# Attention beside early expert tiles: masked queries behind the residual, root between the scatter halves, leaf columns shared anew, keys loaded by quarters, and the last early tile's outputs in three banks

## What is computed

```
attention, per batch and head, over 768 steps t (head_dim 48):
    y[t]   = q[t] @ state
    state += beta[t] * outer(k_n[t], v[t] - k_n[t] @ state)      k_n = k / (|k| + 1e-6)
first expert layer, x of 3072 x 384, 8 experts of 1024:
    P = exp(logits - max), 8 rounds of row and column normalisation
    out += P[:, e] * (relu(x @ w1[e]) @ w2[e])     for every e, all tokens
second layer, 384 -> 2048 -> 384:
    h = x @ w_in;  out = (h * cos(h)) @ w_out
```

## Time and profile before

| | us |
|---|---|
| median of 3 runs | 2282.24 |
| lowest, highest | 2277.13, 2284.86 |
| the profiled execution's own time | 2282.22 |
| its span, first to last instruction | 2280.5 |
| TensorE's mean granted clock | 0.981 |
| attention and early tiles, up to the first matmul of L612 | 393.4 |

### The profile page before, as it was taken

How to read it: one execution, slowest core, us unless ns; L and a number is a source line. 1 busy time by engine, 2 the same in 40 slices (tenths; PEclk the granted TensorE clock), 3 DMA queues, 4 the chain that set the end, 5 groups by cost and what they waited for, 6 DMA issues and landing times.

```text
span 2280.5 us, 40218 instructions
## 1 busy us (share of the span) xinstructions
PE 2222.2 (97%) x15494; PEld 1846.7 (81%) x15494; DVE 1023.6 (45%) x1744; ACT 721.2 (32%) x1153; POOL 508.3 (22%) x404
## 2 busy tenths in 40 slices
PE   4899998999999999999999999999999999999999
PEld 4788786888888888888888888888888888888887
DVE  7787732642222232323232323232323247777777
ACT  4555543311111111111111111111111126666665
POOL 1000001005433333332323232323232331000000
PEclk6799999999999999999999999999999999999999
DMA  5334233202110111111111010111010110000001
GB/s 121 86 86 114 72 102 102 70 16 61 33 32 28 39 35 32 28 32 28 38 35 32 28 32 28 31 42 32 28 33 28 34 36 15 14 14 15 0 15 69
DMA packets 81705, 97.68 MB, mean 43 GB/s; under 512 B 5632, under 2 KB 67392, under 8 KB 81600
## 3 DMA queue, kind: packets, MB, share of 16 engines
q1 hardware_dynamic: 81600, 96.18, 15.7%
HBM read 82.69 MB, written 8.75 MB: 40 GB/s over the span
## 4 chain that ended last, share of the span: by engine, by line
PE 82%; DVE 1%; ACT 0%; issue 0%; DVEq 0%
PE h L612 7%; PE h L613 7%; PE h L614 7%; PE p_h L612 7%; PE p_h L613 7%; PE p_h L614 7%; PE am_y L647 4%; PE am_y L648 4%; PE am_y L649 4%; PE chain_y L647 2%; PE chain_y L648 2%; PE chain_y L649 2%; PE o_y L647 2%; PE state_y L647 2%; PE o_y L648 2%; PE state_y L648 2%
## 5 line engine op out<-in xcount | busy, mean ns | idle before, releaser
L1137 POOL TENSOR_TENSOR acc<-acc,py 128x512 f32 (+1 forms) x252 | 324.3, 1319 | 747.0 <-DVE py L1439 747.0
L1002 ACT ACTIVATE hhi<-h 128x512 fp32r<-128x512 f32 x182 | 109.0, 599 | 769.5 <-PE h L614 769.5
L1402 DVE SCALAR_TENSOR_TENSOR hlo<-h,hhi 128x512 fp32r<-128x512 f32 x182 | 125.9, 692 | 474.6 <-ACT hhi L1002 474.6
L1402 DVE SCALAR_TENSOR_TENSOR hlo<-p_h,hhi 128x512 fp32r<-128x512 f32 x182 | 125.9, 692 | 404.5 <-ACT hhi L1002 404.5
L1099 POOL TENSOR_TENSOR wlo<-stage,whi (+1 forms) x114 | 148.5, 1304 | 652.1 <-ACT whi L881 626.1
L612 PE MATMUL p_h<-xhi,whi 128*128 (+1 forms) x690 | 268.8, 390 | 0.6 <-DVE scr L1499 0.6
L612 PE MATMUL h<-xhi,whi 128*128 (+1 forms) x690 | 268.7, 389 | 0.0
L613 PE MATMUL p_h<-xlo,whi 128*128 (+1 forms) x690 | 268.5, 389 | 0.0
L613 PE MATMUL h<-xlo,whi 128*128 (+1 forms) x690 | 268.4, 389 | 0.0
L614 PE MATMUL p_h<-xhi,wlo 128*128 (+1 forms) x690 | 268.4, 389 | 0.0
L614 PE MATMUL h<-xhi,wlo 128*128 (+1 forms) x690 | 268.4, 389 | 0.0
(11 more groups left out here) (240 smaller groups left out, 3996.7 us busy)
## 6 DMA issues: line engine op xcount, KB each, us to landing
stage<-wcat SPq DMA_DIRECT2D x38, 768.0 KB, 4.3
pb<-p_scratch SPq DMA_DIRECT2D x84, 256.0 KB, 4.7
kq<-kqt SPq DMA_DIRECT2D x48, 192.0 KB, 3.5
kT<-kta SPq DMA_DIRECT2D x24, 192.0 KB, 4.6
v<-vrow SPq DMA_DIRECT2D x24, 192.0 KB, 4.3
kb<-krow SPq DMA_DIRECT2D x24, 192.0 KB, 4.8
acc<-yT SPq DMA_DIRECT2D x72, 64.0 KB, 2.8
acc<-y_scratch SPq DMA_DIRECT2D x5, 768.0 KB, 4.7
```

Of the source, the lines that this page charges most:

```text
L1002: act.activation(hhi[:, j, :], hps[j % 2][:, 0:TILE], ACT.Relu).then_inc(s["hhi_done"], 1)
L1137: pool.tensor_tensor(y, y, py[:, d, :], ALU.add).then_inc(s["added"], 1)
L1402: dve.scalar_tensor_tensor(out=hlo[:, j, :], in0=hps[j % 2][:, 0:TILE], scalar=0.0, in1=hhi[:, j, :].bitcast(F32), op0=ALU.max, op1=ALU.su ...
```

## The change

- `masked(i)` moves from step i-1 to step i, directly behind `residual(i)`. At c=2 and c=3 the leaf and early work is ordered anew: norms and leaf_init of group g+2 come before `early_lo(g-1, 2)`, values of the next step behind it. Columns in steps c=0, 1, 3 change from 12..21 (two lists), 22..30, 1..11 to 10..20, 21..30, 1..9; in group 0 from 4..15, 16..30 (with 1..3 ahead of the loop) to 1..16, 17..30.
- The first three `first_w_lo` move from (g=1, c=0) to (g=1, c=1).
- ACT: `root(g + 2)` is issued between the two halves of `scatter(g + 1, 0)` instead of behind `merged`; scatter walks its elements in the order of the source instead of that of the destination.
- Keys of group 0: eight DMAs of a quarter each, with a semaphore per quarter, in place of four of a half.
- PE prologue: 8 warm matmuls instead of 3; 16 unread matmuls, ahead of the merges, once the leaf chain of group 0 has reached column 27; the waits for zeroed, gate_lo and consts behind the merges.
- DVE prologue: the mask copies ahead of the first extracts; values, masked and the gate's low part behind leaf_end.
- Tail: outputs of tile 4 go to am_ps[0], am_ps[1] and chain_ps; the first of them stands ahead of the logits; `x_hi(NT - 1)` stands ahead of `early_logits(4)` on ACT; `early_lo(4, 3)` ahead of `x_lo(0)` on DVE; the last gate waits for the logits' evacuation only, and the RAW tile's first down product for all of tile 4's.

The diff, cut to its core:

```diff
-COLS = {0: ((12, 14), (14, 22)), 1: ((22, 24), (24, L - 1)), 3: ((), (1, 12))}
-FIRST_COLS = {0: ((4, 7), (7, 16)), 1: ((16, 18), (18, L - 1))}
+COLS = {0: (10, 21), 1: (21, L - 1), 3: (1, 10)}
+FIRST_COLS = {0: (1, 17), 1: (17, L - 1)}
+NEAR_END = 2 + 1 + 2 * 26
...
+    def early_bank(t, d):
+        return (*am_ps, chain_ps)[d] if t == EARLY - 1 else o_ps
...
+        def first_kT(r):
+            for b in range(2):
+                n = slice(r * RU, (r + 1) * RU)
+                at_half = slice(r % 2 * RU * CT, (r % 2 + 1) * RU * CT)
+                sp.dma_start(kT[b * CT:b * CT + HD, n, :].rearrange("p n i -> p (n i)"),
+                             kta[0, r // 2, b, :, at_half]).then_inc(a[f"kt_first{r}"], 16)
...
-        load_kT(0, 0)
-        load_kT(0, 1)
+        for r in range(4):
+            first_kT(r)
...
-            pe.wait_ge(o["evac"], OUTS * t)
+            pe.wait_ge(o["evac"], OUTS * t if t < EARLY else OUTS * (t - 1) + 2)
...
-            pe.wait_ge(o["evac"], OUTS * t + 2 + d)
+            if t < EARLY - 1:
+                pe.wait_ge(o["evac"], OUTS * t + 2 + d)
+            elif d < 2:
+                pe.wait_ge(a["m_evac"], 4 * NG)
+            else:
+                pe.wait_ge(a["w_evac"], NS)
+            bank = early_bank(t, d)
...
-        for _ in range(3):
+        for _ in range(8):
             pe.matmul(p_ps[:, 0:2 * P], stage[:, 0:P], stage[:, P:3 * P], start=True, stop=True)
...
         query_products(0)
+        pe.wait_ge(a["a_evac"], 4)
+        pe.wait_ge(s["whi_done"], 1)
+        pe.wait_ge(a["leaf_chain"], NEAR_END)
+        unread(16)
         for m in range(3):
             merge(0, m)
...
         early_gate(t)
+        early_down(t, 0)
         early_logits(t)
-        for d in range(DC):
-            early_down(t, d)
+        early_down(t, 1)
+        early_down(t, 2)
...
+                if mode == RAW and j == 0:
+                    pe.wait_ge(o["evac"], OUTS * EARLY)
...
-                act.activation(X[L * q:L * q + L, g % 2, n, f:f + L], z_x[L * q:L * q + L, :, n].rearrange("p i n -> p n i"),
+                act.activation(X[L * q:L * q + L, g % 2, n, f:f + L].rearrange("p n i -> p i n"), z_x[L * q:L * q + L, :, n],
...
                 if c >= 2 and near:
-                    scatter(g + 1, c - 2)
+                    scatter(g + 1, c - 2, 0, 2)
+                    if c == 2 and far:
+                        root(g + 2)
+                    scatter(g + 1, c - 2, 2, 4)
                     merged(g + 1, 2 * (c - 2))
-                if c == 2 and far:
-                    root(g + 2)
...
         early_gate(t)
+        x_hi(NT - 1)
         early_logits(t)
         for d in range(DC):
             early_out(t, d)
-        x_hi(NT - 1)
```

More of the change, by code:

```diff
@@ L474, in early_down @@
                 pe.wait_ge(s["wlo_done"], NT)
-            pe.wait_ge(o["evac"], OUTS * t + 2 + d)
+            if t < EARLY - 1:
[5 more added lines that the diff above has]
+            bank = early_bank(t, d)
             for j in range(CH):
-                pe.matmul(o_ps[:, :], w2(whi, 0, j, d), hhi[:, j, :], start=(j == 0), stop=False)
-                pe.matmul(o_ps[:, :], w2(whi, 0, j, d), hlo[:, j, :], start=False, stop=False)
-                mm = pe.matmul(o_ps[:, :], w2(wlo, 0, j, d), hhi[:, j, :], start=False, stop=(j == CH - 1))
+                pe.matmul(bank[:, :], w2(whi, 0, j, d), hhi[:, j, :], start=(j == 0), stop=False)
+                pe.matmul(bank[:, :], w2(whi, 0, j, d), hlo[:, j, :], start=False, stop=False)
+                mm = pe.matmul(bank[:, :], w2(wlo, 0, j, d), hhi[:, j, :], start=False, stop=(j == CH - 1))
             mm.then_inc(o["down_done"], 1)
@@ L586, in _ @@
         pe.wait_ge(a["zeroed"], 2)
-        pe.wait_ge(a["a_evac"], 4)
-        pe.wait_ge(s["whi_done"], 1)
         pe.wait_ge(s["gate_lo"], 1)
@@ L874, in early_out @@
                     act.wait_ge(a["z_done"], NG)
-            act.activation(y_stage(t)[:, d, :], o_ps[:, :], ACT.Copy).then_inc(o["evac"], 1)
+            act.activation(y_stage(t)[:, d, :], early_bank(t, d)[:, :], ACT.Copy).then_inc(o["evac"], 1)
         def split_hi(buf, chunk, p, part=None, came=stage):
@@ L1289, in _ @@
             dve.memset(bank[:, :], 0.0).then_inc(a["zeroed"], 1)
+        dve.wait_ge(a["masks"], 1)
+        for b in range(2):
+            dve.tensor_copy(mask[b * CT:(b + 1) * CT, :], mask_all[b * CT:(b + 1) * CT, b * CT:(b + 1) * CT]).then_inc(a["mask_cut"], 1)
         first_extract(1)
@@ L1294, in _ @@
         leaf_init(0)
-        leaf(1, 12)
+        leaf(1, 28)
+        assert count[0] == NEAR_END
+        leaf(28, L - 1)
+        leaf_end(0)
         values(0)
-        dve.wait_ge(a["masks"], 1)
-        for b in range(2):
-            dve.tensor_copy(mask[b * CT:(b + 1) * CT, :], mask_all[b * CT:(b + 1) * CT, b * CT:(b + 1) * CT]).then_inc(a["mask_cut"], 1)
+        leaf_start(1)
+        dve.wait_ge(a["mask_cut"], 2)
+        masked(0)
+        norms(1)
+        leaf_init(1)
         dve.wait_ge(s["gate_hi"], 1)
@@ L1302, in _ @@
                           ALU.subtract).then_inc(s["gate_lo"], 1)
-        leaf(12, L - 1)
-        leaf_end(0)
-        dve.wait_ge(a["mask_cut"], 2)
-        masked(0)
-        leaf_start(1)
-        norms(1)
-        leaf_init(1)
-        leaf(1, 4)
         for g in range(NG):
@@ L1314, in _ @@
                 i = g * STEPS + c
-                cols = FIRST_COLS if g == 0 and c < 2 else COLS
                 residual(g, c)
-                if c == 2 and g >= 1:
-                    early_x_lo(g - 1)
-                if c == 2 and near:
-                    leaf_end(g + 1)
-                values(i + 1)
+                if i > 0:
+                    masked(i)
                 if c == 0 and g >= 2:
                     early_lo(g - 2, 3)
-                if c == 3 and g >= 1:
-                    early_lo(g - 1, 1)
-                if near and c < 2:
-                    leaf(*cols[c][0])
-                masked(i + 1)
-                if near and c < 2:
-                    leaf(*cols[c][1])
-                if c == 0 and g in (1, 2):
-                    for chunk in range((g - 1) * NT // 2, g * NT // 2):
-                        first_w_lo(chunk)
                 if c == 2:
                     if g >= 1:
+                        early_x_lo(g - 1)
+                    if near:
+                        leaf_end(g + 1)
+                    if g >= 1:
                         early_lo(g - 1, 0)
-                    if far:
-                        leaf_start(g + 2)
                 if c == 3:
                     if g >= 1:
-                        early_lo(g - 1, 2)
+                        early_lo(g - 1, 1)
                     if far:
@@ L1344, in _ @@
                         leaf_init(g + 2)
-                        leaf(*COLS[c][1])
+                    if g >= 1:
+                        early_lo(g - 1, 2)
+                values(i + 1)
+                if c == 2 and far:
+                    leaf_start(g + 2)
+                if near and c < 2:
+                    leaf(*(COLS if g else FIRST_COLS)[c])
+                if far and c == 3:
+                    leaf(*COLS[c])
+                if g == 1 and c == 1 or g == 2 and c == 0:
+                    for chunk in range((g - 1) * NT // 2, g * NT // 2):
+                        first_w_lo(chunk)
+        early_lo(EARLY - 1, 3)
         x_lo(0)
-        early_lo(EARLY - 1, 3)
         x_lo(NT - 1)
```

8 lines of the change are left out of this document (5 added, 3 removed).

## The result

The changed kernel takes 2254.65 us (median of 4 runs, 2252.70 to 2257.68) against 2279.68 (4 runs, 2276.27 to 2284.86) for the kernel before beside it: a ratio of 0.9889, 95% interval 0.9865 to 0.9914. The profiled execution took 2254.29. The prediction was 2255.5, with a range of 2248 to 2266.

A forecast was written before the change was run, and what follows sets the result against it. The prediction took the kernel as PE-bound (busy 97% of 2280.5 us), with the slow clock behind waits as second cost. Ten terms summed to -26.8 us, from a median of 2282.24 to 2255.5, range 2248 to 2266.

The forecast's parts named there:

- Term 1: Prologue: 1.0 us of work leaves DVE's chain, the first transpose comes 0.35 us later: -0.7 us.
- Terms 2 and 3: Step 2: idle for R 1.0 instead of 2.67 us (-1.7); full clock, less 0.6 for z_done (-2.5).
- Rival (b): DVE bounds groups 0 and 1, waits drop the clock, masked shows in two steps: 2262 us, chance 0.21.
- Terms 4 and 5: Step 4: the wait of 3.84 us goes (-3.84) and the step runs at full clock (-3.4).
- The falls behind merges: As many clock falls behind small-matmul merges as before, at 92, 157 and 311 us, some 1.5 us each.
- Rival (a): Unread matmuls carry the clock through step 0, two or three merge falls stay out: 2250 us, chance 0.17.
- Term 6: Steps 4 to 6: small waits as DVE and PE run abreast, 0.5 at step 6's merge: +0.5 us in all.
- Term 7: Step 8's wait of 1.30 us goes; early_down at step 9 waits 1.0 for first_w_lo: -0.3 us.
- Term 8: Step 12's masked comes 0.1 us late; the wait of 0.64 at step 13 goes: -0.5 us.
- term 9: Step 16: the wait of 2.85 us goes with its slow clock, 3.2 us: -6.05 us.
- term 10: Tail: outputs run without bank waits, xlo is ready 3.4 us ahead of its use: -8.3 us.
- Rival (d): Slower: the scatter's strided write on ACT costs more; at 2.5 us each, 2301 us, chance 0.03.

The follow-up runs named there:

- the combined kernel: Changed kernel with first_w_lo ahead of step 8's columns, group 1's column 17 in step 0, three warm and no unread matmuls: 2250.34 us, ratio 0.9868.

## Why the prediction was right

The forecast held, at 2255.5 against 2254.65, and by most of its steps. It was counted from a profile of 2282.22 us, and its 26.8 us stand beside 27.4 at the first up matmul and 27.9 in the spans; between the medians of runs side by side it is 25.0. So the closeness of the two totals, 0.9 us, is in part luck. What each term measured, from the starts of the updates in the table:

| term | forecast | measured |
|---|---|---|
| 1, prologue | -0.7 | -1.5 |
| 2, wait for R at step 2 | -1.7 | -1.8 |
| 3, clock of step 2, less z_done | -2.5 | -2.4 |
| a fall at 92 us that is absent | - | -1.5 |
| 4 and 5, wait and clock of step 4 | -7.2 | -4.0 |
| 6, small waits of steps 5 to 7 | +0.5 | 0, and +1.6 for a fall at 132 us |
| 7, step 8 and wlo | -0.3 | -0.4, and -1.5 for a fall at 157 us that is absent |
| 8, steps 12 and 13 | -0.5 | -0.4 |
| 9, step 16 and its clock | -6.05 | -5.9 |
| a fall at 311 us that is absent | - | -1.6 |
| 10, tail | -8.3 | -8.1 |

**Term 1** had the sign and half the size (0.7 for 1.5). Its DVE part is right: from the first transpose to the first merge it is 33.62 us before, 32.76 after and 32.77 with keys by halves (45.41 less 12.64), 0.9 less where 1.0 was worked out. 0.2 more lie between the first merge and the update. The rest is where the first transpose falls, 0.48 sooner instead of the 0.35 later that I took, within bounds I had given (-1.0 to +0.8) and, by the spread of the profiles, not the change's doing. (At the pace of 0.46 us the 16 halves would end at 8.9, not 8.4; they were through by 7.1.) That eight warm matmuls buy nothing was in the working; that the quarters lose what they bring to them too.

**Terms 2 and 3** are right to a tenth, waits, clock and the new z_done wait each. Rival (b) stood on the 1.0 us wait dropping the clock here; it was 0.91, and the clock was 1.00 behind it.

**Terms 4 and 5** are where the working failed. The wait for R went, as it said. But "step 4 at full clock" did not come: the update of step 4 to that of step 5 takes 12.6 us at a clock of 0.50 from 97.9 on, where 10.2 is the pace of the kernel with the old columns that kept its clock there. I had tied the slow clock of a step to a wait ahead of it. There was none here: PE was busy throughout. The slow stretch itself is not part of the change, since of the eleven experiments with the new list nine don't have it in their profiles at this place; three profiles (the changed kernel, keys by halves, and the combined kernel) do. The same stretch in the kernel without the 16 unread matmuls, columns as above:

```profile
97.90:107.30 9.40, 9.40 (x308) 8.80 (x305) 8.41 (x21) 6.26 (x10) 0.00 (x0) 1.00 0.48 110
```

PE is as busy in both, with 308 matmuls at 1.00 and 190 at 0.50. The price is 3.2 us, 4.0 measured against the 7.2 worked out, all of it between the updates of steps 3 and 5. Of the signs that the prediction named, the clock of 1.00 at step 4 is the one that failed clearly; the first transpose, at 12.92 where 13.0 to 14.2 was named, missed by 0.1.

**The falls behind merges.** I had kept three, 1.5 us each, 4.65 together. All three are absent from their places (92, 157, 311), and two others came: the one in step 4 (3.2 us), and 131.9 to 135.8, 1.6 us (a clock of 0.57 over 3.9 us). That is 4.65 forecast against 4.8: the count was wrong by place and right by price, and that is luck. The other profiles say the same: behind step 0 the kernel with column 17 moved has a single stretch below 1.00 (142 to 148), the one without the unread matmuls three (86 to 90, 160 to 166, 238 to 244). So the three that are absent here are not to the credit of the change. Rival (a), at 2250, needed fewer falls and the full clock in step 0. The second it could not have: the clock is at 0.50 from 50.0 to 63.4 with the unread matmuls, and at 0.50 from 52.7 to 62.2 without.

**Term 6** is not in the changed kernel's profile: no wait of PE lies between 97 and 163 us, as the slow step 4 gave DVE time (the kernels with keys by halves and the combined one, which have that stretch too, have no such small wait there either), and the 1.6 us are the fall at 131.9 (13.81 us from the update of step 6 to that of step 7, against 12.24 in the kernel with x_hi behind the outputs, where the clock holds). Its waits do come where step 4 runs at the full clock, 0.76 us in all in the kernel without the unread matmuls (R 0.17, xlo 0.18, z_done 0.41), and the merge of step 6 is among them as forecast:

```profile
126.50 1.98 PE L447 MATMUL am_y<-stage,A__71 32*32 32x32 f32 x64 [0.41 <-DVE stage L1274]
```

**Term 7** has its new wait, 1.37 us for wlo, within 0.7 to 1.6; the experiment with first_w_lo ahead takes it away and gets 1.0 of it back. **Term 8**, **term 9** and **term 10** are right to 0.25 us. In the tail the slack of x_lo was 4.1 us and not 3.4, and the two experiments split the term: x_hi at its old place gives back 5.8 us, the single bank 3.7. Together that is 1.4 more than the 8.1 of the term. The two overlap: with x_hi at its old place the wait for x_lo is 3.85 us with one bank as with three, and with one bank it covers the gate's own wait for the last evacuation (0.78); behind it the gate's nine matmuls took 3.8 us at three banks and 3.3 at one, by the clock. The prediction's "at most 3.3 us" for a lost cover was too small: 5.8 came back, 3.85 of wait and 2 of slow clock.

**The masked queries** carry half of what the list gained: 10.6 us of medians (ratio 0.9941 against 0.9889, the intervals apart), of which 5.4 are waits, and the rest the clock, by one profile each. The working put what the move buys at c=3, where masked stood ahead of the norms. The experiment leaves the norms ahead and still loses 10.6 us, at steps 1, 2 and 5: wherever masked stands ahead of columns, DVE's wait for the query products delays them. The other half of the list's gain (norms and leaf_init ahead of early_lo, the root between the scatter halves) was not taken apart by an experiment. Rival (b)'s part that masked would show in two steps is false for the changed kernel; it came true where the columns at c=3 are the old ones, once, for 1.8 us at step 12, which is the place that the working named with 0.1. **The new split of the columns** gave nothing that the runs can tell (2254.69 against 2254.65). **Rival (d)** is refuted by the price of the strided write, 1.10 against 1.10.

What stays open: why the clock falls at 97.9 in three profiles and not in the others. The halves or quarters of the keys and the unread matmuls each stood on both sides of it.

## What to carry to other kernels

A wait of several us for a small operation that stands late in another engine's list costs its length and, on TensorE, it cost about as much again here in the clock behind it (3.84 us and 3.4 at step 4, 2.85 and 3.2 at step 16, as the prediction worked out from the profile before). Moving the operation that the other engine needs next to the front of the list, and what has no reader yet behind it, brought 0.8% here without taking any work away. When waits follow one another behind one chain, work out the next one before counting the first as gain: 0.9 us taken away at step 2 left the next wait, 0.58, as it was, because it hangs on the same chain. Where a bank is shared by a row of outputs and other banks are already free, using them takes a wait from each output, and an independent operation put ahead of the outputs hides behind them.

## What the runs showed of the hardware that was not expected

- The granted clock fell to 0.50 with PE 100% busy and no wait ahead: 97.9 to 107.3 in the changed kernel (190 matmul records, all of the stretch busy), at about the same place in two other kernels, and absent in the other nine with the new list. A busy PE by the profile is no assurance of the upper level.
- The clock rose to 1.00 with the 16 unread matmuls and fell again 6 us later, behind the small-matmul merges, for 13.4 us. PE was busy for 4.96 us of the 6.1 ahead of the fall. Warming ahead of such a stretch bought nothing (2254.28 without, 2254.65 with).
- The first transpose moves by over 1 us from profile to profile with nothing ahead of it changed (12.27 to 13.80 with eight warm matmuls). It is the warm matmuls that move it: they let the first key product start at 6.45 to 7.97, and the transpose comes 5.8 us behind that start in all nine profiles. Gains under 1 us in a prologue can't be read from one profile each.
- A strided write of 256 bytes from element to element costs ScalarE what a strided read of 128 bytes does, 1.10 us for 512 elements on 32 partitions. The earlier trace rows shows a form of twice the elements, read in runs of 32, at about the same 1.05, and `y_late` with 512 contiguous elements takes 0.60. The Trainium skill, SBUF — State Buffer, on cachelines, charges an access that crosses to a new line, and the two directions agree with that.
